# Turning the softmax weights of the queries by DMA transposes in place of TensorE transposes

## The chip, the cores and the metric

The kernel runs on one core of a Trainium2 chip. The time is the device time of one execution in microseconds, as the median of several runs; shorter is better. TensorE, VectorE (DVE), ScalarE (ACT), GpSimd (POOL) and the DMA engines work side by side, each following its own list of instructions, and wait for one another on semaphores. SP (SyncE) issues the kernel's DMAs.

## The reference

```python
def _attn_ref(q, k, v, agents):
    scale = 1.0 / np.sqrt(q.shape[-1])
    def sm(a, b):
        s = scale * (a @ b.transpose(0, 2, 1))
        s = s - s.max(-1, keepdims=True)
        e = np.exp(s)
        return e / (e.sum(-1, keepdims=True) + 1e-09)
    agent_v = sm(agents, k) @ v
    return sm(q, agents) @ agent_v          # x, then the layer:

def _moe_ref(x, w_in, w_out, alpha):
    h = x @ w_in
    g = np.maximum(h, 0.0) + alpha * np.minimum(h, 0.0)
    return g @ w_out
```

`q`, `k` and `v` are 2 x 12480 x 128 in float32, `agents` is 2 x 49 x 128, `w_in` 128 x 2048, `w_out` 2048 x 128.

## The kernel before

Setup computes the attention of the 49 agents over the keys and values of batch 0, and folds it with `w_in` into matrices `M_a`, `M_r` (and `L_a`, `L_b` for the linear part of the activation), all float16 in high and low parts. After that, each query needs only its 49 softmax weights: `h` is those weights times the folded matrix.

The main loop goes over 52 chunks of 480 queries, two chunks (`half` 0 and 1) in a body; `n` is the chunk. The bodies come in kinds: KEYS, TOP, VALUES, SUMS, MIX, MIX_REST do pieces of the same setup for batch 1 between the chunks of batch 0, PLAIN bodies (the second half of the run) do nothing beside the chunks. The order of each engine's instructions is written out by hand.

The softmax of chunk n+1 is computed while chunk n is in the second layer. Its parts are:

- TensorE, `query_score` (L501), four float32 matmuls in `second_layer(6)` of the chunk before; DVE, `query_shift`; ACT, `query_exp`; DVE, `query_sum`, `query_norm` (L1096).
- `stack` is 120 queries x 4 tiles x 128 in float16. Columns 0 to 48 are the weights rounded (`query_hi`, ACT L850), the next 49 what the rounding lost (`query_lo`, DVE L1100), the last 30 a copy of part of the high ones (`query_again`, POOL L354).
- `query_turn` (TensorE L517): four transposes, 120 x 128 to 128 x 120, into the PSUM bank `SMALL`; they stand behind the two `linear` matmuls of chunk n (L551). `query_out` (ACT L854) copies the result to `PT`, 128 x 480.
- `spread` (SP L259): rows 0 to 31 of `PT` are copied to rows 32 to 63, 64 to 95 and 96 to 127 of `PR` by three DMAs of 30 KB.

Both buffers have a half for each parity of n. A chunk then is, on TensorE: `tiles(p)` (L524), two matmuls `PT` x `M_a` of 480 columns for each of eight pairs p of feature tiles; `rest_of_quad(q)` (L531), four matmuls of 32 rows on `PT` and `PR` for each two pairs; and `second_layer(p)` (L541), six matmuls. ACT makes `r_hi` (`relu_hi`, L862) of each pair from the PSUM, DVE makes `r_lo` (`relu_lo`, L1105). `tiles(p)` waits for the low part of the pair that had its PSUM slot before (three slots). `tiles(0)`, `tiles(1)` and `rest_of_quad(0)` of chunk n+1 stand before `second_layer(6)` of chunk n, and `rest_of_quad(0)` is the first that waits for `PR`:

```python
tiles(0, 1 - half, nb)
pe.wait_ge(lo_ready, g + 7)
tiles(1, 1 - half, nb)

pe.wait_ge(q_spread, 48 * n + 96)
rest_of_quad(0, 1 - half, nb)
```

SP's list in one chunk of a PLAIN body: the load of `q` for chunk n+2 (L276), the three copies into `PR`, the store of `y` (L295). In KEYS and VALUES bodies a load of 512 or 768 KB into `kv_s` (L280, L289) stands before the copies.

Of the kernel before, what the change touches and what calls it, by code (L numbers as in the profile page):

```python
# [6 lines left out]
F16 = mybir.dt.float16  # L7
ALU = mybir.AluOpType
# [6 lines left out]
T = 120  # L15
CHUNK = 4 * T
CHUNKS = B * N // CHUNK
KT = 128
# [22 lines left out]
def build(nc, kT, kTail, vP, vS, vTail, qT, agT, w_inT, w_out, alpha_col, out):  # L41
    ctx = ExitStack()
    with ctx:
# [8 lines left out]
        ident16 = sb("ident16", [128, 128], F16)  # L52
# [85 lines left out]
        def slot(p):  # L138
# [14 lines left out]
        consts, pool_step, dve_step = sem("consts"), sem("pool_step"), sem("dve_step")  # L153
# [17 lines left out]
        q_scored, q_maxed, q_shifted, q_exped, q_summed, q_dened, q_reced, q_normed, q_hi, q_lo, q_turned, q_ready, q_dup, q_spread = (  # L171
            sem(x) for x in ("q_scored", "q_maxed", "q_shifted", "q_exped", "q_summed", "q_dened", "q_reced",
                             "q_normed", "q_hi", "q_lo", "q_turned", "q_ready", "q_dup", "q_spread"))
# [48 lines left out]
        def _(sp):  # L222
# [38 lines left out]
            spread(0, 0)  # L261
# [8 lines left out]
            def body(i, b, kind, last):  # L270
                for half in range(2):
                    n = 2 * i + half
                    if not last:

                        sp.wait_ge(q_scored, n + 1)
                        sp.dma_start(q_s[:, half, :], qT[n + 2]).then_inc(in_q[half], 16)  # L276
                    if kind == KEYS and (not isinstance(n, int) or n + 2 + EARLY <= FULL):

                        sp.wait_ge(k_scored, n + (FULL + EARLY + 2))
                        sp.dma_start(kv_s[:, half, :], kT[1, n + (EARLY + 1)]).then_inc(in_k[half], 16)  # L280
                    if kind == TOP:

                        sp.wait_ge(v_used, FULL + 1)
                        sp.dma_start(second_s[:, half * SECOND * C:(half + 1) * SECOND * C],
                                     vS[half]).then_inc(in_second[half], 16)
                    if kind == VALUES and (not isinstance(n, int) or n + 2 - FIRST_VALUES < SECONDS):

                        sp.wait_ge(v_used, n + (FULL + 2 - FIRST_VALUES))
                        sp.dma_start(second_s[:, half * SECOND * C:(half + 1) * SECOND * C],  # L289
                                     vS[n + (2 - FIRST_VALUES)]).then_inc(in_second[half], 16)  # L290
                    if not (last and half == 1):
                        spread(n + 1, 1 - half)
# [9 lines left out]
        def _(pool):  # L302
            pool.memset(agents[:, B * A:128], 0.0).then_inc(consts, 1)
            pool.memset(ident[:, :], 0.0).then_inc(pool_step, 1)
            pool.memset(ident16[:, :], 0.0).then_inc(pool_step, 1)
# [5 lines left out]
            pool.wait_ge(pool_step, 3)  # L311
            for m in (ident, ident16):
                pool.affine_select(out=m[:, :], in_=m[:, :], compare_op=ALU.not_equal, fill=1.0, base=0,
                                   pattern=[[-1, 128]], channel_multiplier=1).then_inc(consts, 1)
# [3 lines left out]
            steps = 3  # L318
# [23 lines left out]
            pool.wait_ge(consts, 8)  # L342
# [8 lines left out]
            def query_again(n):  # L351

                pool.wait_ge(q_hi, n + 1)
                pool.tensor_tensor(stack[:, :, 2 * A:128], stack[:, :, REST:A],  # L354
                                   ones[0:T, 0:4 * SPARE].rearrange("p (t a) -> p t a", a=SPARE), ALU.mult).then_inc(q_dup, 1)
# [29 lines left out]
        def _(pe):  # L385
# [124 lines left out]
            def query_turn(n):  # L510

                pe.wait_ge(q_hi, n + 1)
                pe.wait_ge(q_lo, n + 1)
                pe.wait_ge(q_dup, n + 1)
                turned = ps[:, SMALL, :].bitcast(F16)
                for t in range(4):
                    mm = pe.transpose(turned[:, t * T:(t + 1) * T], stack[:, t, :], ident16[0:T, 0:T])  # L517
                mm.then_inc(q_turned, 1)


            def tiles(p, half, b):
                for u in range(2):
                    f = 128 * (2 * p + u)
                    pe.matmul(ps[:, 2 * slot(p) + u, 0:CHUNK], M_a[:, b, f:f + 128], PT[:, half, :],  # L524
                              start=True, stop=False)


            def rest_of_quad(q, half, b):
                for u in range(4):
                    src = PT if u == 0 else PR  # L530
                    mm = pe.matmul(ps[:, 2 * slot(2 * q + u // 2) + u % 2, 0:CHUNK],  # L531
                                   M_r[32 * u:32 * u + 32, b, q * 128:(q + 1) * 128],
                                   src[32 * u:32 * u + 32, half, :], start=False, stop=True)
                mm.then_inc(h_ready, 1)
# [14 lines left out]
            def linear(half, b):  # L549
                for w, end in ((L_a, False), (L_b, True)):  # L550
                    mm = pe.matmul(ps[:, 2 * LIN_SLOT, 0:CHUNK], w[:, b, :], PT[:, half, :], start=not end, stop=end)  # L551
                mm.then_inc(lin_ready, 1)
# [5 lines left out]
            for m in range(1, FULL + 1):  # L558
                first_scores(m)
                if m == 7:  # L560

                    pe.wait_ge(consts, 8)
                    relu_max_row()
                if m == 8:
                    relu_max_everywhere()
# [26 lines left out]
            query_turn(0)  # L592
# [8 lines left out]
            pe.wait_ge(q_ready, 1)  # L601
# [21 lines left out]
            pe.wait_ge(m_low, 1)  # L623
            tiles(0, 0, 0)
# [11 lines left out]
            def body(i, b, kind, last):  # L636
                for half in range(2):
# [85 lines left out]
                    if ahead:  # L723

                        if keys:
                            pe.wait_ge(k_saved, n + (FULL + EARLY + 2))
                        if kind == TOP and half == 1:
                            pe.wait_ge(b_shift, 2)
                        if kind == VALUES:
                            pe.wait_ge(av_added, n + (1 - FIRST_VALUES))  # L730
                        if kind == SUMS and half == 0:
                            pe.wait_ge(av_added, SECONDS + 1)
                        if kind == SUMS and half == 1:
                            pe.wait_ge(b_dened, 2)
                        if kind == MIX:
                            pe.wait_ge(m_low, 5 + 2 * half)
                        if kind == MIX_REST and half == 0:
                            pe.wait_ge(r_low, 2)
                        query_turn(n + 1)

# [7 lines left out]
                    if ahead:  # L748
                        pe.wait_ge(q_ready, n + 2)
                    if kind == TOP and half == 0:  # L750
                        key_max_rows(1, SMALL)
                    if kind == SUMS and half == 1:
                        value_sums(1, SMALL)
                    if kind == MIX:
                        mix(1, 2 * half + 1, SMALL)
                    if kind == MIX_REST and half == 0:
                        mix_linear(1, SMALL)
                    second_layer(5, half)

                    if ahead:  # L760
                        pe.wait_ge(lin_saved, n + 1)
                        if kind == MIX_REST and half == 1:
                            pe.wait_ge(m_low, 8)
                            pe.wait_ge(r_low, 2)
                            pe.wait_ge(l_low, 2)
                        tiles(0, 1 - half, nb)
# [8 lines left out]
                    else:  # L775
                        pe.wait_ge(in_q[half], 16 * i + 32)

                        if kind == TOP and half == 0:
                            pe.wait_ge(b_diag, 2)
                        if kind == SUMS and half == 1:  # L780
                            pe.wait_ge(b_vmax, 2)
# [18 lines left out]
        def _(act):  # L800
# [47 lines left out]
            def query_hi(n):  # L848
                act.wait_ge(q_normed, n + 1)
                act.activation(stack[:, :, 0:A], q_p[:, :, :], ACT.Copy).then_inc(q_hi, 1)  # L850
# [18 lines left out]
            for m in range(FULL + 1):  # L869
# [11 lines left out]
                if m == 11:  # L881
                    query_out(0, 0)
# [15 lines left out]
            def body(i, b, kind, last):  # L898
                for half in range(2):
# [20 lines left out]
                    if ahead:  # L920
                        query_out(n + 1, 1 - half)
# [27 lines left out]
        def _(dve):  # L949
# [148 lines left out]
            def query_lo(n):  # L1098
                dve.wait_ge(q_hi, n + 1)
                dve.tensor_tensor(stack[:, :, A:2 * A], q_p[:, :, :], stack[:, :, 0:A], ALU.subtract).then_inc(q_lo, 1)  # L1100
# [12 lines left out]
            dve.wait_ge(consts, 8)  # L1113
# [169 lines left out]
```

## Time and profile before

| | us |
|---|---|
| median of 3 runs | 944.13 (944.05 to 944.71) |
| the profiled execution | 944.28 |
| its span in the profile | 942.8 |

| engine | busy, share of the span | instructions |
|---|---|---|
| TensorE matmuls | 925.7 us (98%) | 5850 |
| TensorE weight loads | 499.9 (53%) | 5850 |
| DVE | 635.4 (67%) | 926 |
| ACT | 540.4 (57%) | 746 |
| POOL | 109.1 (12%) | 142 |

The span is what the profiler's records cover, the time is the whole execution, 1.5 us more. A TensorE matmul is listed with its own duration, 0.37 us for 480 columns, and the next starts 0.2 us after it, since they are pipelined: the distance between starts is what one costs. The granted clock is 1.00 at TensorE's full 2.4 GHz and 0.50 at 1.2 GHz.

### The profile page before, as it was taken

Reading aid. Unit: us, or ns where it says so; the run is one execution under the profiler, and the core shown is the slowest. Engines: PE = TensorE matmul, PEld = TensorE weight load, DVE = VectorE, ACT = ScalarE, POOL = GpSimd, SP = SyncE. Lnnn points to the kernel's source line nnn. Section 1 sums busy time; section 2 is a strip of 40 time slices with the busy share of each in tenths; the row PEclk is TensorE's granted clock in tenths of the full one; section 3 lists DMA queues with packets and bytes.
Section 4 is the critical chain, followed back from the end, with each engine's and each line's share of the span. In section 5 each row is a group of like instructions: output and inputs, shape, how many; then the busy total and the mean of one; then the engine's idle time right before and its main releaser. Section 6 shows DMA issues by size and latency. Waiting matters only on the chain.

```text
span 942.8 us, 16143 instructions
## 1 busy us (share of the span) xinstructions
PE 925.7 (98%) x5850; PEld 499.9 (53%) x5850; DVE 635.4 (67%) x926; ACT 540.4 (57%) x746; POOL 109.1 (12%) x142
## 2 busy tenths in 40 slices
PE   7899999999999999999999999999999999999998
PEld 7784555555546556554444444444444444444443
DVE  4567666666767767767776676766666666666664
ACT  2236565565565565565656666666666666656564
POOL 6220100101001001001001010101010101010101
PEclk9799999999999999999999999999999999999999
DMA  8650221221212311201101110101111110101010
GB/s 296 262 189 28 62 77 51 77 64 48 80 63 70 102 62 66 72 29 46 29 26 47 29 46 29 46 29 45 30 43 32 36 39 32 42 26 47 26 37 24
DMA packets 29922, 58.55 MB, mean 62 GB/s; under 512 B 5248, under 2 KB 24000, under 8 KB 29632
## 3 DMA queue, kind: packets, MB, share of 16 engines
q1 hardware_dynamic: 29600, 58.03, 18.9%
q8 instruction: 23, 0.38, 0.2%
q14 instruction: 11, 0.09, 0.0%
q10 hardware_dynamic: 288, 0.06, 0.0%
HBM read 40.49 MB, written 12.78 MB: 57 GB/s over the span
## 4 chain that ended last, share of the span: by engine, by line
PE 94%; DVE 2%; issue 2%; DMA 1%; ACT 1%; SPq 0%; POOLq 0%; ACTq 0%
PE ps L541 54%; PE ps L524 17%; PE ps L531 7%; PE ps L501 3%; PE ps L551 2%; PE ps L388 2%; PE ps L694 2%; PE ps L688 1%; PE ps L517 1%; PE ps L464 1%; DMA kv_s<-kT 1%; PE ps L412 1%; PE ps L482 1%; DVE r_lo L1105 0%; PE ps L419 0%
## 5 line engine op out<-in xcount | busy, mean ns | idle before, releaser
L1105 DVE SCALAR_TENSOR_TENSOR r_lo<-ps,r_hi 128x960 f16<-128x960 f32 x416 | 466.5, 1153 | 259.4 <-ACT r_hi L862 256.7
L862 ACT ACTIVATE r_hi<-ps 128x960 f16<-128x960 f32 x416 | 386.3, 967 | 154.3 <-PE ps L531 149.2
L541 PE MATMUL ps<-r_hi,w_hi 128*128 128x480 f16 x832 | 252.1, 369 | 0.3 <-DVE M_a L1057 0.3
L541 PE MATMUL ps<-r_hi,w_lo 128*128 128x480 f16 x832 | 248.1, 366 | 0.0
L541 PE MATMUL ps<-r_lo,w_hi 128*128 128x480 f16 x832 | 240.7, 366 | 0.0
L524 PE MATMUL ps<-PT,M_a 128*128 128x480 f16 x832 | 204.0, 366 | 0.7 <-DVE r_lo L1105 0.7
L373 POOL TENSOR_TENSOR y<-y_relu,y_lin 128x480 f32<-128x480 f32 x52 | 62.4, 1200 | 627.4 <-issue 377.3
L541 PEld LDWEIGHTS ps<-r_hi,w_lo 128*128 128x128 f16 x832 | 91.4, 111 | 68.5
L541 PEld LDWEIGHTS ps<-r_lo,w_hi 128*128 128x128 f16 x832 | 85.4, 106 | 71.0
L541 PEld LDWEIGHTS ps<-r_hi,w_hi 128*128 128x128 f16 x832 | 77.1, 106 | 86.0 <-issue 41.9
L524 PEld LDWEIGHTS ps<-PT,M_a 128*128 128x128 f16 x832 | 75.6, 98 | 80.1 <-DVE r_lo L1105 16.8
L531 PE MATMUL ps<-PR,M_r 32*128 32x480 f16 x624 | 78.6, 371 | 0.0
L531 PE MATMUL ps<-PT,M_r 32*128 32x480 f16 x208 | 77.3, 372 | 0.2 <-DMA PR<-PT 0.2
L501 PEld LDWEIGHTS ps<-agents,q_s 128*120 128x120 f32 x416 | 71.2, 187 | 3.9
L943 ACT ACTIVATE y_relu<-ps,out_unscale 128x480 f32<-128x480 f32 x52 | 34.4, 662 | 65.2 <-PE ps L541 65.2
L854 ACT ACTIVATE PT<-ps 128x480 f16<-128x480 f16 x52 | 29.7, 571 | 64.7 <-PE ps L517 64.7
L501 PE MATMUL ps<-agents,q_s 128*120 128x49 f32 x416 | 65.0, 241 | 0.0
L531 PEld LDWEIGHTS ps<-PT,M_r 32*128 32x128 f16 x208 | 18.9, 91 | 82.9 <-issue 81.4
L850 ACT ACTIVATE stack<-q_p 120x196 f16<-120x196 f32 x52 | 19.4, 373 | 60.4 <-DVE q_p L1096 60.4
L354 POOL TENSOR_TENSOR stack<-stack,ones 120x120 f16<-120x120 f16 x52 | 20.9, 402 | 179.2 <-ACT stack L850 179.2
L926 ACT ACTIVATE y_lin<-ps,lin_unscale 128x480 f32<-128x480 f32 x52 | 34.1, 656 | 1.1 <-PE ps L551 1.1
L694 PEld LDWEIGHTS ps<-S,kv_s 128*128 128x128 f32 x192 | 33.2, 190 | 1.4
(146 smaller groups left out, 599.6 us busy)
## 6 DMA issues: line engine op xcount, KB each, us to landing
q_s<-qT SPq DMA_DIRECT2D x52, 240.0 KB, 2.6
out<-y SPq DMA_DIRECT2D x52, 240.0 KB, 2.0
kv_s<-kT SPq DMA_DIRECT2D x24, 512.0 KB, 4.4
kv_s<-vP SPq DMA_DIRECT2D x12, 512.0 KB, 6.7
kv_s<-vS SPq DMA_DIRECT2D x8, 768.0 KB, 4.4
PR<-PT SPq DMA_DIRECT2D x156, 30.0 KB, 1.9
w_lin<-w_out SPq DMA_DIRECT2D x1, 1024.0 KB, 6.8
w_inT_s<-w_inT SPq DMA_DIRECT2D x1, 1024.0 KB, 5.6
```

Source lines behind the costliest of these rows:

```text
L354: pool.tensor_tensor(stack[:, :, 2 * A:128], stack[:, :, REST:A], ones[0:T, 0:4 * SPARE].rearrange("p (t a) -> p t a", a=SPARE), ALU.mult) ...
L373: pool.tensor_tensor(y[:, half, :], y_relu[:, half, :], y_lin[:, half, :], ALU.add).then_inc(y_ready, 1)
L501: return pe.matmul(ps[0:T, SMALL, t * A:(t + 1) * A], q_s[:, half, t * T:(t + 1) * T], agents[:, b * A:(b + 1) * A], start=True, stop=True)
L524: pe.matmul(ps[:, 2 * slot(p) + u, 0:CHUNK], M_a[:, b, f:f + 128], PT[:, half, :], start=True, stop=False)
L531: mm = pe.matmul(ps[:, 2 * slot(2 * q + u // 2) + u % 2, 0:CHUNK], M_r[32 * u:32 * u + 32, b, q * 128:(q + 1) * 128], src[32 * u:32 * u + ...
L541: mm = pe.matmul(ps[:, OUT, 0:CHUNK], w[:, 2 * p + u, :], r[:, s, u, :], start=(p == 0 and u == 0 and k == 0), stop=(p == PAIRS - 1 and u ...
L694: mm = pe.matmul(ps[:, SMALL, 0:A], second_s[:, at:at + C], S[:, 1, SECOND * n + (t + 2 - SECOND * FIRST_VALUES), :], start=(t == 0), stop ...
L854: act.activation(PT[:, half, :], ps[:, SMALL, :].bitcast(F16)[:, 0:CHUNK], ACT.Copy).then_inc(q_ready, 1)
L862: act.activation(r_hi[:, p % RING, :, :], ps[:, at:at + 2, 0:CHUNK], ACT.Relu).then_inc(hi_ready, 1)
L926: act.activation(y_lin[:, half, :], ps[:, 2 * LIN_SLOT, 0:CHUNK], ACT.Copy, scale=lin_unscale[:, b, :]).then_inc(lin_saved, 1)
L943: act.activation(y_relu[:, half, :], ps[:, OUT, 0:CHUNK], ACT.Copy, scale=out_unscale[:, b, :]).then_inc(relu_saved, 1)
L1105: dve.scalar_tensor_tensor(out=r_lo[:, p % RING, :, :], in0=ps[:, at:at + 2, 0:CHUNK], scalar=0.0, in1=r_hi[:, p % RING, :, :], op0=ALU.ma ...
```

## The change

The four TensorE transposes of a chunk, their PSUM output and the copy to `PT` on ACT are gone. SP issues four DMA transposes of 128 x 128 from `stack` to `PT`, waits for them to land, and then issues the three copies to `PR`. For this `stack` gets 128 partitions (the last 8 are zeroed once, by one memset on the DVE), and `PT` and `PR` get 512 columns for each half, of which 120 in each 128 are used; the matmuls on them read them in four runs. The float16 identity is gone from POOL's list. The waits that stood before `query_turn` for the PSUM bank move to where the bank is used next. TensorE waits for the transposes before `tiles(0)` of the next chunk.

```diff
-        stack = sb("stack", [T, 4, 128], F16)
-        PT = sb("PT", [128, 2, CHUNK], F16)
-        PR = sb("PR", [128, 2, CHUNK], F16)
+        stack = sb("stack", [WIDE, 4, 128], F16)
+        PT = sb("PT", [128, 2, 4 * WIDE], F16)
+        PR = sb("PR", [128, 2, 4 * WIDE], F16)
...
-            def spread(n, half):
-
-                sp.wait_ge(q_ready, n + 1)
+            def turn(n, half):
+
+                sp.wait_ge(stack_zero, 1)
+                sp.wait_ge(q_hi, n + 1)
+                sp.wait_ge(q_dup, n + 1)
+                sp.wait_ge(q_lo, n + 1)
+                for t in range(4):
+                    sp.dma_start(PT[:, half, t * WIDE:(t + 1) * WIDE], stack[:, t, :], transpose=True).then_inc(q_turned, 16)
+
+                sp.wait_ge(q_turned, 64 * n + 64)
                 for g in range(32, 128, 32):
                     sp.dma_start(PR[g:g + 32, half, :], PT[0:32, half, :]).then_inc(q_spread, 16)
...
-            def query_turn(n):
-
-                pe.wait_ge(q_hi, n + 1)
-                pe.wait_ge(q_lo, n + 1)
-                pe.wait_ge(q_dup, n + 1)
-                turned = ps[:, SMALL, :].bitcast(F16)
-                for t in range(4):
-                    mm = pe.transpose(turned[:, t * T:(t + 1) * T], stack[:, t, :], ident16[0:T, 0:T])
-                mm.then_inc(q_turned, 1)
+            def tokens(x, half):
+                return x[:, half, :].rearrange("p (t n) -> p t n", n=WIDE)[:, :, 0:T]
...
-                    pe.matmul(ps[:, 2 * slot(p) + u, 0:CHUNK], M_a[:, b, f:f + 128], PT[:, half, :],
+                    pe.matmul(by_tile(ps[:, 2 * slot(p) + u, 0:CHUNK]), M_a[:, b, f:f + 128], tokens(PT, half),
                               start=True, stop=False)
...
+                        pe.wait_ge(q_turned, 64 * n + 128)
+                        tiles(0, 1 - half, nb)
+                        pe.wait_ge(lo_ready, g + 7)
+                        tiles(1, 1 - half, nb)
+
+                        pe.wait_ge(q_spread, 48 * n + 96)
+                        rest_of_quad(0, 1 - half, nb)
...
-            def query_out(n, half):
-                act.wait_ge(q_turned, n + 1)
-                act.activation(PT[:, half, :], ps[:, SMALL, :].bitcast(F16)[:, 0:CHUNK], ACT.Copy).then_inc(q_ready, 1)
...
+            dve.memset(stack[:, :, :], 0.0).then_inc(stack_zero, 1)
```

In the loop over the PLAIN bodies, TensorE's list between `linear` and `second_layer(4)` was this; L551 is `linear`, L517 the transposes, L524 `tiles(6)` and `tiles(7)`, L531 `rest_of_quad(3)`:

```order
L551 MATMUL ps<-PT,L_b 128x480
L512 REGISTER_ALU
L517 MATMUL ps<-ident,stack 128x120 [waits q_dup,q_lo,q_hi]
L517 MATMUL ps<-ident,stack 128x120 x3
L741 REGISTER_ALU
L524 MATMUL ps<-PT,M_a 128x480 [waits lo_ready]
L524 MATMUL ps<-PT,M_a 128x480
L743 REGISTER_ALU
L524 MATMUL ps<-PT,M_a 128x480 [waits lo_ready]
L524 MATMUL ps<-PT,M_a 128x480
L531 MATMUL ps<-PT,M_r 128x480
```

and is this in the changed kernel, whose lines are numbered five higher or more (L556 is `linear`, L529 `tiles`, L536 `rest_of_quad`):

```order
L556 MATMUL ps<-PT,L_b 128x480
L729 REGISTER_ALU
L529 MATMUL ps<-PT,M_a 128x480 [waits lo_ready]
L529 MATMUL ps<-PT,M_a 128x480
L731 REGISTER_ALU
L529 MATMUL ps<-PT,M_a 128x480 [waits lo_ready]
L529 MATMUL ps<-PT,M_a 128x480
L536 MATMUL ps<-PT,M_r 128x480
```

The transposes and their wait for `stack` are gone from between `linear` and `tiles(6)`; nothing else moved there. SP's list for one chunk of the same loop was this:

```order
L276 ISA [waits q_scored]
L276 DMA q_s<-qT 128x480
L259 DMA PR<-PT 32x480 [waits q_ready]
L259 DMA PR<-PT 32x480 x2
L295 ISA [waits y_ready]
L295 DMA out<-y 128x480
```

and is now this:

```order
L286 ISA [waits q_scored]
L286 DMA q_s<-qT 128x480
L265 DMA_TRANSPOSE PT<-stack 128x128 [waits q_dup,q_lo,q_hi,stack_zero]
L265 DMA_TRANSPOSE PT<-stack 128x128 x3
L267 ISA
L269 DMA PR<-PT 32x512 [waits q_turned]
L269 DMA PR<-PT 32x512 x2
L305 ISA [waits y_ready]
L305 DMA out<-y 128x480
```

Four transposes and a wait for them stand ahead of the copies, which began on ACT's copy before.

## Rows read from the trace of the kernel before

**Rows 1.** Busy time by stretch: stretch, its length, each engine's, PEclk, DMA share.

```profile
698.94:714.82 15.88, 15.88 (x95) 7.60 (x95) 10.77 (x16) 9.74 (x13) 1.60 (x2) 1.00 0.12 37
```

**Rows 2.** Waits of TensorE, whole run: who, for whom, us in total, times, longest.

```profile
PE ps L531 <- DMA PR<-PT: 0.2, 1, 0.2
```

**Rows 3.** Timeline, last stage: start, us, instructions; then idle before and its releaser.

```profile
698.94 0.37 PE L531 MATMUL ps<-PT,M_r 32*128 32x480 f16 x1
...
707.93 0.35 DVE L1100 TENSOR_TENSOR stack<-q_p,stack 120x196 f16<-120x196 f32 x1
```

**Rows 4.** Timeline, same chunk, from the end of `stack` to `rest_of_quad(0)`.

```profile
708.37 2.22 DVE L1105 SCALAR_TENSOR_TENSOR r_lo<-ps,r_hi 128x960 f16<-128x960 f32 x2
...
710.01 0.38 PE L517 MATMUL ps<-ident,stack 120*128 120x120 f16 x4
...
710.23 1.00 PE L524 MATMUL ps<-PT,M_a 128*128 128x480 f16 x4
710.43 0.57 ACT L854 ACTIVATE PT<-ps 128x480 f16<-128x480 f16 x1 [1.23 <-PE ps L517]
710.64 0.11 PEld L524 LDWEIGHTS ps<-PT,M_a 128*128 128x128 f16 x2 [0.32 <-DVE r_lo L1105]
...
711.02 1.78 SPq L259 DMA_DIRECT2D PR<-PT  x3
...
713.92 0.97 PE L524 MATMUL ps<-PT,M_a 128*128 128x480 f16 x4
...
714.82 0.37 PE L531 MATMUL ps<-PT,M_r 32*128 32x480 f16 x1
```

**Rows 5.** The copies into `PR`: issue min/median/max ns, first and last start; landing.

```profile
L259 SPq DMA_DIRECT2D PR<-PT x156: 512/590/1503, 60.6 to 918.7; - x156
...
DMA to landing us min/median/max: 1.8/1.9/2.8
```

**Rows 6.** Timeline, a chunk of the KEYS stage with a slow issue.

```profile
226.03 2.71 SPq L259 DMA_DIRECT2D PR<-PT  x3
...
230.06 0.09 PEld L531 LDWEIGHTS ps<-PT,M_r 32*128 32x128 f16 x1 [0.67 <-DMA PR<-PT]
```

**Rows 7.** Timeline, last stage: the load of `q` on the SP queue.

```profile
705.30 0.35 SPq L276 DMA_DIRECT2D q_s<-qT  x1
```

**Rows 8.** Timeline of KEYS, VALUES and SUMS: the end of `stack`, `rest_of_quad(0)`.

```profile
136.11 0.35 DVE L1100 TENSOR_TENSOR stack<-q_p,stack 120x196 f16<-120x196 f32 x1
...
144.24 0.37 PE L531 MATMUL ps<-PT,M_r 32*128 32x480 f16 x1
...
325.76 0.35 DVE L1100 TENSOR_TENSOR stack<-q_p,stack 120x196 f16<-120x196 f32 x1
325.77 0.33 SPq L289 DMA_DIRECT2D kv_s<-vS  x1
...
334.31 0.37 PE L531 MATMUL ps<-PT,M_r 32*128 32x480 f16 x1
...
432.08 0.35 DVE L1100 TENSOR_TENSOR stack<-q_p,stack 120x196 f16<-120x196 f32 x1
...
439.23 0.37 PE L531 MATMUL ps<-PT,M_r 32*128 32x480 f16 x1
```

**Rows 9.** The value loads of 768 KB (L289): time to landing.

```profile
DMA to landing us min/median/max: 4.1/4.3/4.4
```

**Rows 10.** Busy time by stretch around two pauses of TensorE in the setup.

```profile
19.50:21.50 2.00, 0.06 (x2) 0.05 (x2) 2.00 (x2) 0.50 (x1) 0.00 (x0) 1.00 0.89 297
21.50:24.90 3.40, 3.40 (x15) 2.98 (x16) 0.97 (x3) 0.00 (x0) 0.00 (x0) 0.50 0.40 154
...
62.90:64.30 1.40, 0.15 (x3) 0.07 (x1) 1.18 (x3) 0.00 (x0) 0.00 (x0) 1.00 0.47 116
65.90:69.30 3.40, 3.40 (x23) 3.04 (x19) 1.48 (x5) 0.52 (x2) 0.00 (x0) 0.50 0.98 355
```

More of the change, by code:

```diff
@@ L291, in body @@
                     if not (last and half == 1):
-                        spread(n + 1, 1 - half)
+                        turn(n + 1, 1 - half)
                     sp.wait_ge(y_ready, n + 1)
@@ L310, in _ @@
             pool.memset(av_acc[:, :], 0.0).then_inc(consts, 1)
[L311 to L314, printed above, removed]
+            pool.wait_ge(pool_step, 2)
+            pool.affine_select(out=ident[:, :], in_=ident[:, :], compare_op=ALU.not_equal, fill=1.0, base=0,
+                               pattern=[[-1, 128]], channel_multiplier=1).then_inc(consts, 1)
             pool.affine_select(out=gate[:, :], in_=gate[:, :], compare_op=ALU.is_ge, fill=0.0, base=-2 * A,
                                pattern=[[0, 1]], channel_multiplier=1).then_inc(consts, 1)
-            steps = 3
+            steps = 2
             def then(instruction):
@@ L353, in query_again @@
                 pool.wait_ge(q_hi, n + 1)
[L354 removed]
+                pool.tensor_tensor(stack[0:T, :, 2 * A:128], stack[0:T, :, REST:A],
                                    ones[0:T, 0:4 * SPARE].rearrange("p (t a) -> p t a", a=SPARE), ALU.mult).then_inc(q_dup, 1)
@@ L530, in rest_of_quad @@
                     src = PT if u == 0 else PR
-                    mm = pe.matmul(ps[:, 2 * slot(2 * q + u // 2) + u % 2, 0:CHUNK],
+                    mm = pe.matmul(by_tile(ps[:, 2 * slot(2 * q + u // 2) + u % 2, 0:CHUNK]),
                                    M_r[32 * u:32 * u + 32, b, q * 128:(q + 1) * 128],
-                                   src[32 * u:32 * u + 32, half, :], start=False, stop=True)
+                                   tokens(src[32 * u:32 * u + 32, :, :], half), start=False, stop=True)
                 mm.then_inc(h_ready, 1)
@@ L550, in linear @@
                 for w, end in ((L_a, False), (L_b, True)):
-                    mm = pe.matmul(ps[:, 2 * LIN_SLOT, 0:CHUNK], w[:, b, :], PT[:, half, :], start=not end, stop=end)
+                    mm = pe.matmul(by_tile(ps[:, 2 * LIN_SLOT, 0:CHUNK]), w[:, b, :], tokens(PT, half), start=not end,
+                                   stop=end)
                 mm.then_inc(lin_ready, 1)
@@ L722, in body @@
                     linear(half, b)
[L723 to L739, printed above, removed]
                     pe.wait_ge(lo_ready, g + 5)
@@ L746, in body @@
                     second_layer(4, half)
-                    if ahead:
-                        pe.wait_ge(q_ready, n + 2)
                     if kind == TOP and half == 0:
+                        pe.wait_ge(k_saved, 2 * FULL + 2)
                         key_max_rows(1, SMALL)
                     if kind == SUMS and half == 1:
+                        pe.wait_ge(b_dened, 2)
                         value_sums(1, SMALL)
                     if kind == MIX:
+                        pe.wait_ge(m_low, 5 + 2 * half)
                         mix(1, 2 * half + 1, SMALL)
                     if kind == MIX_REST and half == 0:
+                        pe.wait_ge(r_low, 2)
                         mix_linear(1, SMALL)
@@ L776, in body @@
                         pe.wait_ge(in_q[half], 16 * i + 32)
+                        if kind == KEYS:
+                            pe.wait_ge(k_saved, n + (FULL + EARLY + 2))
                         if kind == TOP and half == 0:
                             pe.wait_ge(b_diag, 2)
+                        if kind == TOP and half == 1:
+                            pe.wait_ge(b_shift, 2)
+                        if kind == VALUES:
+                            pe.wait_ge(av_added, n + (1 - FIRST_VALUES))
+                        if kind == SUMS and half == 0:
+                            pe.wait_ge(av_added, SECONDS + 1)
                         if kind == SUMS and half == 1:
@@ L1099, in query_lo @@
                 dve.wait_ge(q_hi, n + 1)
-                dve.tensor_tensor(stack[:, :, A:2 * A], q_p[:, :, :], stack[:, :, 0:A], ALU.subtract).then_inc(q_lo, 1)
+                dve.tensor_tensor(stack[0:T, :, A:2 * A], q_p[:, :, :], stack[0:T, :, 0:A], ALU.subtract).then_inc(q_lo, 1)
             def relu_lo(g, p):
```

29 lines of the change are left out of this document (13 added, 16 removed).

## The prediction

> **What bounds the kernel now.** I read the busy shares by stretch first. Over one chunk of the last stage TensorE is busy for all of its 15.88 us, at the full granted clock [rows 1], and in the whole run it waits for the copies in `PR` just once, for 0.2 us [rows 2]. So any time that TensorE gets back is worth something, and any time for which it is made to wait is a loss. What decides is therefore the two things that the change touches: the TensorE work of the transposes, and the slack of the path that brings the turned weights to TensorE.
>
> For that path I followed one chunk of the last stage in order of time. `rest_of_quad(0)` of one chunk starts at 698.94, the score matmuls for the next one follow, then its softmax, woven on the DVE between the low parts of this chunk; the last piece of `stack` ends at 707.93 + 0.35 = 708.28 [rows 3]. From 698.94 to there is **9.34 us**. All of it follows from `rest_of_quad(0)` through work that the change leaves alone, so this length stays. From 708.28 to the next `rest_of_quad(0)` at 714.82 [rows 4] is **6.54 us**: the budget of everything between `stack` and `PR`. The sum of the two is the period of 15.88 us.
>
> **What the change removes.** Four transposes on TensorE: from 710.01 to the next matmul at 710.23 [rows 4], 0.22 us per chunk, 52 x 0.22 = 11.4 us if all of it came back (the 0.38 us of the four overlap with their neighbours, so the distance of starts is the price). It does not come back. Two matmuls further, the third `L524` of the group is `tiles(7)`, which needs the fourth low part of the DVE, and the DVE's two operations run 708.37 to 708.37 + 2.22 = 710.59, with the weight load at 710.64 already waiting for them [rows 4]. They follow from `rest_of_quad(2)` through ScalarE (`relu_hi`), not from the transposes, which come later on TensorE. Without transposes TensorE stands there 0.2 us earlier and waits until 710.64 all the same. What is left is the 0.03 us by which that group of four takes 1.00 instead of the 0.97 of its like at 713.92 [rows 4]. I take the removal at **0 us**, with 0.03 x 52 = 2 us as its most in the last stage and, in the others, at most the 0.1 or so between these times. The PSUM copy was 0.57 us on ScalarE beside TensorE's work [rows 4], a gain of 0 by itself.
>
> The wider buffers (512 columns in place of 480 in each copy), the single DVE memset at the start and the one memset and one select fewer on GpSimd I take at 0: TensorE's first long wait ends at 21.5 [rows 10] and is for `w_col`, long after them. The matmuls read `PT` in four runs of 120 columns with a gap; no row shows such a read, it is the same count of columns, and I take 0. If each run cost a few ns on the 8 or so matmuls of the 9.34 us, that is under 0.2 us per chunk, inside the range below.
>
> **What the change adds.** Before, the path from `stack` to `PR` was: turn and copy, with `PT` ready at 711.00, then three copies issued from 711.02 [rows 4]. The issue of one takes 0.52 to 0.59 us, it lands 1.9 us after its issue began [rows 5]; the third starts 1.19 us after the first (1.78 - 0.59). So `PR` is there at 711.02 + 1.19 + 1.9 = 714.11 against a need at 714.82: 0.7 us of slack. That the landing is rightly read shows where an issue was slow: three issues took 2.71 us from 226.03, the third began at 226.03 + 2.71 - 0.59 = 228.15, + 1.9 = 230.05, and TensorE's load is released at 230.06 [rows 6].
>
> Now the SP queue issues four transposes after `stack`, waits until the last has landed, and only then issues the three copies. Two DMAs thus stand in series where before there was one. With an issue price i and a landing l of a transpose, the path is
>
> W = 0.02 + 3i + l + 0.02 + 1.19 + 1.9 + 0.04 = 3.17 + 3i + l,
>
> where 0.02 is the SP's start after its release (711.00 to 711.02) and 0.04 TensorE's start after a landing, rounded up. If W is over a chunk's budget, the excess is TensorE idle time, and the period is 9.34 + W. Behind the waiting SP stands only the store of `y`, released some 9 us later, so nothing else is queued behind that wait; behind TensorE's wait stands everything.
>
> No row shows a transposing DMA. The bounds: i not under the 0.35 us of a plain load of 128 rows, not over the 1.503 us of the slowest issue of a copy; l from 1.8 to 2.8 us, the extremes of the copies [rows 5, 7]. The nearest row is the plain copy within the SBUF, 0.59 and 1.9. A transpose has four times its rows, and spreads elements of two bytes over partitions, so I hold that it costs more than this and not less; I take the middle of the bounds, **i = 0.93, l = 2.3, W = 8.26 us**.
>
> The budgets of the other stages, from the end of `stack` to `rest_of_quad(0)` [rows 8]: chunks with a key piece 144.24 - 136.46 = 7.78 (9 like it); with values 334.31 - 326.11 = 8.20 (9 like it; there a 768 KB load is issued at 325.77, 0.34 us ahead of the transposes, and lands after 4.3 us [rows 9], so they may queue behind it; with 3i + l = 5.1 they end after it anyway); seven chunks at the seams between 6.8 and 7.8, mean 7.15, of which the shortest kind is 439.23 - 432.43 = 6.80; and the last stage's 6.54, 26 times. Together 51; the first chunk's turn lies in the setup, where the copies were issued at 60.6 [rows 5], well ahead of the loop.
>
> Sum: 26 x (8.26 - 6.54) = 44.7; 7 x (8.26 - 7.15) = 7.8; 9 x 0.48 = 4.3; 9 x 0.06 = 0.5; together **57 us**, all of it TensorE waiting for `PR`. The profiled execution took 944.28 us (the median of the runs is 944.13, so the two can be taken as one), which gives **1001 us**. By the same formula the nearest row's prices (W = 6.84) give 26 x 0.30 = 8, so 952 us; the upper bounds (W = 10.47) give 102 + 23 + 24 + 20 = 169, so 1114 us; the lower bounds (W = 6.02) give no wait at all.
>
> The Trainium skill weighs in on both sides. Its page "Advanced Engine Details and Errata" (X-Bar Transpose (TRN2)) says that transposing DMAs are as fast as regular ones; by that it would be the 952 us case. Its page "VectorE: DVE Perf Modes" (The three transpose paths) gives 1309 ns for a 128x128 transpose by DMA; an estimate with that as i and 2.3 as l gives W = 9.4 and some 1060 us. No row here tells between them.
>
> **The rivals.** *A. The DMAs are cheap, the path fits (not slower).* It decides at W = 6.54: with l = 1.9 that needs i under 0.49, so a transpose that issues faster than the plain copy, at most like the 0.35 us load. For it: such an issue exists in the trace, for a load [rows 7]. Against: all copies within the SBUF took at least 0.51. Then only the gain remains, which the DVE holds to 0 to 4 us: 940 to 944 us. If the DVE did not hold it, it would be 933 us; the row at 710.64 [rows 4] speaks against that.
>
> *B. The waits bring TensorE's clock down.* After TensorE had stood still for 1.94 us in 19.50 to 21.50, its granted clock was 0.5, 1.2 GHz, for the next 3.4 us; after a pause of 1.25 us at 63 to 64.3 the same came over 65.9 to 69.3 [rows 10]. Such a stretch costs half its length, 1.7 us. In the forecast TensorE pauses for 1.7 us in each chunk of the last stage. 33 chunks with it (26 and 7) would add 56 us, all 51 would add 87: 1057 to 1088 us. Against it: around those two pauses TensorE ran small float32 matmuls, while in the last stage dense float16 work would stand on both sides of each pause, as nowhere in this trace. That pauses lower the clock is also what the Trainium skill says ("TensorE: Matmul & The Clock Gate", on oscillation in real kernels), and the trace agrees that it can happen.
>
> *C. The transposes are dearer than every bound here*, since 2-byte elements are moved one by one: beyond 1114 us, each further us of W costs 51.
>
> That the transposes stay on TensorE is no rival: in the order of the changed kernel they are gone from the engine and stand in the SP queue.
>
> **How the numbers follow.** Forecast (W over the budget, clock full, up to 1114): 0.70, point 1001. B: 0.12. C: 0.05. A: 0.13, of which same 0.08 and faster 0.05. A change of about 0.2% (1.9 us) is what can be told from none. Slower is 0.70 + 0.12 + 0.05 = 0.87. The range goes from the nearest row's 952, less 4 for a gain at `tiles(7)`, that is 948, up to the bounds' 1114: it leaves out A, C and little of B, somewhat under 0.2.
>
> **What would show it.** Right: in the last stage a period of 17.6 us; TensorE idle 1.7 us before `rest_of_quad(0)`, released by the copies into `PR`; SP waiting for the transposes; issues of about 0.9 us each; `tiles(7)` waiting 0.2 us for `r_lo`. No `L524` waits for `PT` itself, as the transposes are to land 5.1 us after `stack` and `tiles(0)` stands at about 5.4. Wrong: a period of 15.7 (A without the DVE), TensorE's clock below full in the last stage (B), or matmuls on `PT` longer than 0.37 us.

## The result and the profile after

The changed kernel takes **1110.85 us** (median of 4 runs, 1108.26 to 1113.56) against 944.09 of the kernel before (4 runs): a ratio of 1.177, 95% interval 1.173 to 1.180. It is slower, as forecast, and inside the range; but the point of 1001 us stood for a loss of 57 us, and the loss is 167 us, about three times that. The profiled execution took 1108.89 us, its span is 1107.2.

The line of TensorE on the page after, and its waits over the whole run (who, for whom, us in total, times, longest), which answer to [rows 2]:

```profile
PE 977.6 (88%) x5642; PEld 509.8 (46%) x5642; DVE 635.7 (57%) x927; ACT 516.2 (47%) x694; POOL 108.8 (10%) x140
```

```profile
PE ps L536 <- DMA PR<-PT: 95.6, 51, 3.3
...
PE ps L529 <- DMA PT<-stack: 14.4, 31, 0.8
```

TensorE stood still for 0.2 us for `PR` before; now it does in each of the 51 chunks that are turned in the loop, 95.6 us in all, and for `PT` 14.4 us more. That is 110 us. The matmuls were busy for 925.7 us before and for 977.6 now, though there are 208 fewer of them: 52 us more. Both are lost time, and the second is not a wait: most of it is the clock, as the rows below show.

One chunk of the last stage, in order of time, from one `rest_of_quad(0)` (L536) to the next; these rows answer to [rows 3] and [rows 4] (start, us, instructions; idle before and its releaser):

```profile
880.95 0.37 PE L536 MATMUL ps<-PT,M_r 32*128 32x480 f16 x1 [2.14 <-DMA PR<-PT]
...
883.54 1.00 PE L546 MATMUL ps<-r_hi,w_hi 128*128 128x480 f16 x2
...
884.34 1.00 PE L546 MATMUL ps<-r_hi,w_lo 128*128 128x480 f16 x2
...
887.20 0.58 PE L546 MATMUL ps<-r_hi,w_hi 128*128 128x480 f16 x2
...
891.62 0.35 DVE L1092 TENSOR_TENSOR stack<-q_p,stack 120x196 f16<-120x196 f32 x1
...
892.07 4.95 SPq L265 DMA_TRANSPOSE PT<-stack  x4
...
893.71 1.21 PE L529 MATMUL ps<-PT,M_a 128*128 128x480 f16 x4
...
894.34 0.11 PEld L529 LDWEIGHTS ps<-PT,M_a 128*128 128x128 f16 x2 [0.53 <-DVE r_lo L1097]
...
898.21 1.81 SPq L269 DMA_DIRECT2D PR<-PT  x3
...
898.24 0.98 PE L529 MATMUL ps<-PT,M_a 128*128 128x480 f16 x4 [0.47 <-DMA PT<-stack]
...
901.33 0.37 PE L536 MATMUL ps<-PT,M_r 32*128 32x480 f16 x1 [2.10 <-DMA PR<-PT]
```

The period is 901.33 - 880.95 = 20.38 us, where it was 15.88. From the end of `stack` (891.97) to `rest_of_quad(0)` it is 9.36 us; that was 6.54. The other piece, from `rest_of_quad(0)` to the end of `stack`, is 11.02 us and was 9.34, and here nothing waits for a DMA. Two matmuls of the second layer take 1.00 us from 883.54 on and 0.58 from 887.20 on: the clock. The busy times by stretch (stretch, length, each engine's, PEclk, DMA share), beside [rows 1]:

```profile
880.95:901.33 20.38, 17.74 (x91) 7.80 (x92) 10.77 (x15) 9.28 (x12) 1.60 (x2) 0.92 0.13 35
882.53:885.94 3.41, 3.41 (x11) 1.38 (x10) 2.79 (x4) 0.77 (x1) 0.00 (x0) 0.51 0.00 0
```

For 3.4 us, from 1.6 us after the pause on, TensorE's granted clock is half, 1.2 GHz, and the chunk loses 11.02 - 9.34 = 1.68 us there. Of the 26 chunks of the last stage 23 look like this, with periods of 20.34 us and up, and 3 keep the full clock and have 18.6 to 18.7, which is 9.36 + 9.34; outside that stage four chunks have the fall.

The DMAs, beside [rows 5] (issue min/median/max in ns, first and last start; landing):

```profile
L265 SPq DMA_TRANSPOSE PT<-stack x208: 1107/1232/1892, 54.1 to 1077.6; - x104
...
DMA to landing us min/median/max: 2.3/2.4/4.6
```

A transpose keeps the SP queue for 1.23 us, twice the 0.59 of a plain copy, and lands 2.4 us after its issue began.

Both parts in one sum, on the profiled executions (1108.89 - 944.28 = 164.6 us): with W = 9.36 in the prediction's formula the waits come to 26 x 2.82 + 7 x 2.21 + 9 x 1.58 + 9 x 1.16 = 113 us; the clock to 27 x 1.67 = 45 us; 6 us remain, of which a few slow issues make some 3 (in the last chunk W is 10.8).

### The profile page after: what moved, and what is told of

It is laid out like the page before. It is cut to its first block, busy times and chain, and to the rows that moved or that the text cites. A ratio compares the mean times of both kernels' runs of the same rounds, so it can differ in the third digit from the quotient of the medians.

```text
span 1107.2 us, 15981 instructions
## 1 busy us (share of the span) xinstructions
PE 977.6 (88%) x5642; PEld 509.8 (46%) x5642; DVE 635.7 (57%) x927; ACT 516.2 (47%) x694; POOL 108.8 (10%) x140
## 4 chain that ended last, share of the span: by engine, by line
PE 33%; SPq 22%; DMA 21%; DVE 14%; issue 5%; ACT 4%; POOLq 0%; ACTq 0%
PE ps L546 17%; SPq L265 17%; DMA PT<-stack 11%; DMA PR<-PT 9%; DVE r_lo L1097 7%; SPq L269 5%; ACT r_hi L858 4%; PE ps L529 4%; PE ps L509 4%; PE ps L536 3%; PE ps L396 2%; DVE stack L1092 1%; PE ps L700 1%; DVE q_sum L1080 1%; PE ps L472 1%
## 5 line engine op out<-in xcount | busy, mean ns | idle before, releaser
L546 PE MATMUL ps<-r_hi,w_hi 128*128 128x480 f16 x832 | 264.9, 385 | 0.3 <-DVE M_a L1049 0.3
L546 PE MATMUL ps<-r_hi,w_lo 128*128 128x480 f16 x832 | 263.5, 385 | 0.0
L546 PE MATMUL ps<-r_lo,w_hi 128*128 128x480 f16 x832 | 254.2, 384 | 0.0
L529 PE MATMUL ps<-PT,M_a 128*128 128x480 f16 x832 | 211.8, 367 | 17.5 <-DMA PT<-stack 14.4
L536 PE MATMUL ps<-PT,M_r 32*128 32x480 f16 x208 | 77.6, 373 | 95.6 <-DMA PR<-PT 95.6
L529 PEld LDWEIGHTS ps<-PT,M_a 128*128 128x128 f16 x832 | 74.8, 99 | 125.1 <-DVE r_lo L1097 28.0
L546 PEld LDWEIGHTS ps<-r_hi,w_lo 128*128 128x128 f16 x832 | 97.0, 117 | 74.5 <-issue 10.3
L546 PEld LDWEIGHTS ps<-r_lo,w_hi 128*128 128x128 f16 x832 | 90.2, 112 | 74.5 <-issue 6.2
L546 PEld LDWEIGHTS ps<-r_hi,w_hi 128*128 128x128 f16 x832 | 80.6, 110 | 94.3 <-issue 58.5
L536 PEld LDWEIGHTS ps<-PT,M_r 32*128 32x128 f16 x208 | 18.8, 91 | 181.7 <-DMA PR<-PT 119.3
L509 PEld LDWEIGHTS ps<-agents,q_s 128*120 128x120 f32 x416 | 88.1, 228 | 7.6
L536 PE MATMUL ps<-PR,M_r 32*128 32x480 f16 x624 | 79.0, 373 | 0.0
L509 PE MATMUL ps<-agents,q_s 128*120 128x49 f32 x416 | 77.5, 278 | 0.0
L694 PEld LDWEIGHTS ps<-agents,kv_s 128*128 128x128 f32 x176 | 30.9, 191 | 1.1
```

Of the source, the lines that this page charges most:

```text
L509: return pe.matmul(ps[0:T, SMALL, t * A:(t + 1) * A], q_s[:, half, t * T:(t + 1) * T], agents[:, b * A:(b + 1) * A], start=True, stop=True)
L529: pe.matmul(by_tile(ps[:, 2 * slot(p) + u, 0:CHUNK]), M_a[:, b, f:f + 128], tokens(PT, half), start=True, stop=False)
L536: mm = pe.matmul(by_tile(ps[:, 2 * slot(2 * q + u // 2) + u % 2, 0:CHUNK]), M_r[32 * u:32 * u + 32, b, q * 128:(q + 1) * 128], tokens(src[ ...
L546: mm = pe.matmul(ps[:, OUT, 0:CHUNK], w[:, 2 * p + u, :], r[:, s, u, :], start=(p == 0 and u == 0 and k == 0), stop=(p == PAIRS - 1 and u ...
```

## The experiments

The theory at this point: (1) only the length of the path from `stack` to `PR` makes TensorE wait, and the issues of the four transposes make it long; (2) TensorE's pauses bring its clock down, and that is 45 of the 165 us; (3) the 0.22 us of the TensorE transposes would not come back even if the waits were gone, since the DVE's low part holds `tiles(7)`. The rivals are named with each run.

### Plain copies in place of the transposes

```diff
-                    sp.dma_start(PT[:, half, t * WIDE:(t + 1) * WIDE], stack[:, t, :], transpose=True).then_inc(q_turned, 16)
+                    sp.dma_start(PT[:, half, t * WIDE:(t + 1) * WIDE], stack[:, t, :]).then_inc(q_turned, 16)
```

> The changed kernel with four plain copies of the same tiles in place of the four DMA transposes (PT then holds untransposed data, so the output is not the reference's); every wait stays. Theory (the issue price of a transpose on the SP queue, 1.24 us each, is what lengthens the path from stack to PR): issues fall to 0.59 us, landing to 1.9, the path from 9.36 to about 6.9 us, TensorE waits some 0.3 us per chunk of the last stage, its clock stays full: about 952 us. Rival 1 (two DMA steps in series cost this much whatever they are): near 1100. Rival 2 (the clock falls because of the missing TensorE transposes, not because of the pause): the path is short but the clock still falls in most chunks, about 995.

Measured: 956.45 us (ratio 1.013, 1.011 to 1.015). The SP queue and the wait at `rest_of_quad(0)` in the last stage:

```profile
810.87 2.45 SPq L265 DMA_DIRECT2D PT<-stack  x4
814.62 1.82 SPq L269 DMA_DIRECT2D PR<-PT  x3
```

```profile
801.43 0.37 PE L536 MATMUL ps<-PT,M_r 32*128 32x480 f16 x1 [0.38 <-DMA PR<-PT]
...
817.76 0.37 PE L536 MATMUL ps<-PT,M_r 32*128 32x480 f16 x1 [0.39 <-DMA PR<-PT]
```

Four issues take 2.45 us where the transposes took 4.95, and the period is 817.76 - 801.43 = 16.33. Two DMA steps in series cost 12 us; that the first of them is made of transposes costs the other 155, with the clock that falls behind the longer pauses. In the loop of this run the clock is full.

### Half of the transposes

```diff
-                for t in range(4):
+                for t in range(2):
                     sp.dma_start(PT[:, half, t * WIDE:(t + 1) * WIDE], stack[:, t, :], transpose=True).then_inc(q_turned, 16)
 
-                sp.wait_ge(q_turned, 64 * n + 64)
+                sp.wait_ge(q_turned, 32 * n + 32)
```

TensorE's waits for the transposes are halved in the same way, and the DVE zeroes `PT` once at the start.

> The changed kernel with two transposes per chunk in place of four (the other half of PT stays zero, so the output is not the reference's). Theory: two issues of 1.24 us less, the path is 9.36 - 2.48 = 6.88 us, the clock stays full: about 953 us. Rival (the price is in the landing of a transpose, or in the wait, not in the issue of each): the path stays over 8 us, and the time over 1000.

Measured: 953.52 us (ratio 1.010, 1.008 to 1.012).

```profile
809.89 2.40 SPq L265 DMA_TRANSPOSE PT<-stack  x2
813.48 1.81 SPq L269 DMA_DIRECT2D PR<-PT  x3
```

```profile
816.62 0.37 PE L536 MATMUL ps<-PT,M_r 32*128 32x480 f16 x1 [0.22 <-DMA PR<-PT]
```

From the first issue of the transposes to the first of the copies is now 813.48 - 809.89 = 3.59 us; with four it was 898.21 - 892.07 = 6.14. Two issues of 1.2 us less shorten the path by 2.55: the price is in the issue of each, not in the landing or the wait as such.

### Work in the pause

```diff
                         tiles(1, 1 - half, nb)
+                        if kind == PLAIN:
+                            for _ in range(14):
+                                pe.matmul(ps[:, SMALL, 200:500], w_hi[:, 0, :], M_a[:, 1, 0:300], start=True, stop=True,
+                                          skip_group_check=True)
```

> The changed kernel with 14 added matmuls of 300 columns into unused columns of the PSUM bank SMALL, in each chunk of the last stage, between tiles(1) and the wait for PR; the output is not changed. They fill about 1.8 of the 2.1 us of pause. Theory (the pauses bring the clock down, and each fall costs 1.67 us in about 23 chunks of the last stage): the period of the last stage is 18.7 in place of 20.4 us, the clock full there: about 1072 us. Rival 1 (the clock falls whatever TensorE does in the pause): 1111 us. Rival 2 (added work delays rest_of_quad(0)): over 1111.

Measured: 1072.68 us (ratio 1.136, 1.133 to 1.139), 38 us less than the changed kernel, with more work in it. The filler and the wait behind it, then two stretches of the last stage in this run:

```profile
933.89 1.95 PE L763 MATMUL ps<-M_a,w_hi 128*128 128x300 f16 x14
...
936.20 0.37 PE L536 MATMUL ps<-PT,M_r 32*128 32x480 f16 x1 [0.36 <-DMA PR<-PT]
...
954.89 0.37 PE L536 MATMUL ps<-PT,M_r 32*128 32x480 f16 x1 [0.32 <-DMA PR<-PT]
```

```profile
900.00:950.00 50.00, 48.14 (x279) 22.88 (x278) 30.15 (x44) 26.30 (x36) 4.79 (x6) 1.00 0.14 41
950.00:1000.00 50.00, 47.45 (x281) 23.58 (x279) 28.33 (x41) 23.88 (x31) 4.39 (x5) 1.00 0.13 37
```

and the same two of the changed kernel:

```profile
900.00:950.00 50.00, 43.35 (x232) 21.05 (x232) 26.52 (x40) 23.13 (x30) 4.40 (x5) 0.93 0.13 37
950.00:1000.00 50.00, 43.47 (x222) 19.93 (x218) 27.31 (x36) 23.25 (x30) 3.60 (x5) 0.93 0.13 36
```

The clock goes from 0.93 to 1.00, and the path to `PR` is as long as before: the period is 954.89 - 936.20 = 18.69 us, as in the chunks of the changed kernel that kept the clock. So the pause is what brings the clock down, and 38 us is what that cost in the last stage: 23 chunks by 1.67.

### The same path made of plain copies

```diff
+                for t in range(4):
+                    sp.dma_start(again[:, t * WIDE:(t + 1) * WIDE], stack[:, t, :]).then_inc(q_again, 16)
                 for t in range(4):
-                    sp.dma_start(PT[:, half, t * WIDE:(t + 1) * WIDE], stack[:, t, :], transpose=True).then_inc(q_turned, 16)
+                    sp.dma_start(PT[:, half, t * WIDE:(t + 1) * WIDE], stack[:, t, :]).then_inc(q_turned, 16)
```

> The run plain with four more plain copies of the stack, into a buffer that nobody reads, issued ahead of the four copies into PT (the output is not the reference's). No transposing DMA is in it. By the formula the path from stack to PR is 3.2 + 7 x 0.61 + 1.9 = 9.4 us, as with the transposes. Theory (only the length of the path counts, for the waits and for the clock): the same 1105 to 1115 us, the granted clock at half for 3.4 us in most chunks of the last stage. Rival (the fall of the clock belongs to the transposing DMAs): the waits as expected, the clock full: 1060 to 1070 us.

Measured: 1131.7 us (ratio 1.200, 1.197 to 1.204): 17 us above the theory's 1105 to 1115 and 21 above the changed kernel, and far from the rival's.

```profile
826.62 2.45 SPq L267 DMA_DIRECT2D again<-stack  x4
829.12 2.53 SPq L269 DMA_DIRECT2D PT<-stack  x4
832.92 1.83 SPq L274 DMA_DIRECT2D PR<-PT  x3
```

```profile
832.95 0.98 PE L534 MATMUL ps<-PT,M_a 128*128 128x480 f16 x4 [0.62 <-DMA PT<-stack]
...
836.03 0.56 PE L541 MATMUL ps<-PT,M_r 32*128 32x480 f16 x1 [2.10 <-DMA PR<-PT]
```

```profile
900.00:950.00 50.00, 44.40 (x230) 21.15 (x230) 27.62 (x42) 23.26 (x32) 4.79 (x6) 0.92 0.16 44
```

From the first issue to the copies it is 6.30 us, 0.16 more than with the transposes, and the first pause 0.62 in place of 0.47. The clock falls without any transposing DMA. That a path of nearly the same length costs 21 us more lies partly in its 0.16 us (51 x 0.16 = 8 us), partly in the clock, which falls in all 26 chunks of the last stage here and in more chunks ahead of it. The mean granted clock is 0.939 over a span of 1127.5 us, and 0.949 over 1107.2 in the changed kernel, so that 0.061 x 1127.5 - 0.051 x 1107.2 = 12 us more are lost to it. Why it falls in more chunks was not tried.

This run also has pauses that leave the clock up. In the key stage TensorE waits for `PR` alone, 1.7 us in each of the six chunks from 156.23 to 269.39 us, and the clock stays full there (the wait of one chunk, then the stretch of all six, with PEclk 1.00):

```profile
212.91 0.37 PE L541 MATMUL ps<-PT,M_r 32*128 32x480 f16 x1 [1.71 <-DMA PR<-PT]
```

```profile
156.23:269.39 113.16, 102.70 (x636) 56.18 (x638) 70.11 (x97) 57.91 (x78) 9.60 (x12) 1.00 0.24 69
```

In the changed kernel these chunks have pauses of 1.5 to 1.6 us, also at full clock.

### TensorE never waits for the DMAs

TensorE reads the first chunk's weights from buffers of their own, and all DMAs are issued as before; ScalarE waits for a chunk's copies before it writes `stack` anew, which TensorE's reads assured before:

```diff
-                    pe.matmul(by_tile(ps[:, 2 * slot(p) + u, 0:CHUNK]), M_a[:, b, f:f + 128], tokens(PT, half),
+                    pe.matmul(by_tile(ps[:, 2 * slot(p) + u, 0:CHUNK]), M_a[:, b, f:f + 128], tokens(PT0, half),
...
-                        pe.wait_ge(q_turned, 64 * n + 128)
...
-                        pe.wait_ge(q_spread, 48 * n + 96)
```

> The changed kernel, all transposes and copies issued as before, but TensorE reads the weights of the first chunk for every chunk, from buffers of their own, and so never waits for the DMAs of the loop (the output is not the reference's). Theory (the DVE's low parts hold tiles(7), so TensorE gets back almost nothing of the 0.22 us of transposes per chunk): 940 to 944 us, with a wait of about 0.2 us for r_lo before tiles(7) in each chunk of the last stage. Rival (TensorE's work is the only bound): 944 - 11 = 933 us, and no such wait. If the reads of PT in four runs cost something, the matmuls of tiles stand further apart than 0.203 us.

Measured: 943.05 us (10 runs; ratio 0.9986, 0.9977 to 0.9996). The chunk around `tiles(7)`:

```profile
802.72 1.21 PE L532 MATMUL ps<-PT,M_a 128*128 128x480 f16 x4
...
806.62 0.97 PE L532 MATMUL ps<-PT,M_a 128*128 128x480 f16 x4
```

```profile
803.35 0.11 PEld L532 LDWEIGHTS ps<-PT,M_a 128*128 128x128 f16 x2 [0.53 <-DVE r_lo L1100]
```

The group with `tiles(7)` takes 1.21 us, 0.24 more than its like, and the load waits for `r_lo`: 0.21 us longer than in [rows 4]. The 0.22 us of the transposes have become this wait. The other group, also read from four runs of 120 columns, takes 0.97 us as before, so that read costs nothing. And the DMAs, all in flight, disturb nobody.

### Two matmuls ahead of the wait

```diff
+                    second_layer(4, half, part=(0,))
                     pe.wait_ge(lo_ready, g + 6)
                     tiles(7, half, b)
                     rest_of_quad(3, half, b)
-                    second_layer(4, half)
+                    second_layer(4, half, part=(1, 2))
```

This on top of the run free, and alone on the kernel before:

> The run free (TensorE reads the first chunk's weights throughout and never waits for the DMAs of the loop; the output is not the reference's), with the first two matmuls of second_layer(4) moved ahead of tiles(7). Theory (the DVE's low part of pair 5 is what kept the 0.22 us of the transposes per chunk from coming back in free, where a wait of that length stood before tiles(7)): the two matmuls fill it, the period of the last stage falls from 15.86 to 15.66 us, and the time from 943 to about 933 us. Rival (the time in free is set by something else, such as the reads of PT in four runs): 943 us again.

> The kernel before, with only the move of the two matmuls of second_layer(4) ahead of tiles(7). TensorE had no wait there but 0.03 us, as its transposes filled the time: 942 to 944 us, no difference to speak of. If the move by itself saves time, it is below 940.

Measured: 932.08 us (ratio 0.987, 0.986 to 0.989) with it on free, 943.99 us (11 runs; ratio 1.000, 0.999 to 1.001) on the kernel before. The move is worth nothing by itself and 11 us once the transposes are off TensorE. Work taken away and the wait behind it have to go together.

### The turn one chunk earlier

The whole softmax of the queries runs one chunk further ahead; the transposes of chunk n+2 wait until TensorE has read the same half of `PT` for the last time in chunk n:

```diff
-                sp.wait_ge(q_hi, n + 1)
                 sp.wait_ge(q_dup, n + 1)
                 sp.wait_ge(q_lo, n + 1)
+                if not (isinstance(n, int) and n < 2):
+                    sp.wait_ge(pt_free, n + 1)
...
-                    if not (last and half == 1):
-                        turn(n + 1, 1 - half)
+                    if not last:
+                        turn(n + 2, half)
```

and likewise `query_shift`, `query_exp`, `query_sum`, `query_norm`, `query_hi`, `query_lo` and `query_again` of n+2 for n+1, and the scores and the load of chunk n+3 for n+2. ACT waits for the transposes before it writes `stack` anew.

> The changed kernel with the whole softmax of the queries, its DMA transposes and copies one chunk earlier against their use: chunk n+2 is turned while chunk n runs, once TensorE has done with the same half of PT; the output is the reference's. Theory (only the length of the path from stack to PR, 9.4 us against a budget of 6.5, made the change slow, and with it the clock): no wait for PT or PR in any chunk, full clock, and the time of the run free, 943 us, with 1 to 2 us more in the setup: 942 to 946. Rival (the DMAs disturb other work, or the SP queue becomes late): over 950.

> The run deep with the first two matmuls of second_layer(4) ahead of tiles(7); the output is the reference's. Theory: both gains of the change come out, 933 to 937 us, about 1% under the kernel before. Rival (the wait for r_lo only moves elsewhere): 943 us.

Measured: deep 948.7 us (9 runs; ratio 1.004, 1.003 to 1.005), above the expected 946; deep_early 939.01 us (5 runs; ratio 0.995, 0.993 to 0.996), above the expected 937. No chunk of the loop waits for `PT` or `PR` any more. What was missed lies in the setup: the first chunk of deep took 24.67 us between the first two `rest_of_quad(0)`, 18.33 before, for this:

```profile
80.21 0.36 DVE L1099 TENSOR_TENSOR q_e<-ps,q_top 120x196 f32<-120x196 f32 x1
...
80.83 0.56 PE L556 MATMUL ps<-r_hi,w_hi 128*128 128x480 f16 x1 [2.91 <-DVE q_e L1099]
```

The third softmax's shift stood behind a low part on the DVE, and TensorE waited 2.91 us for it before its first `second_layer`; the matmuls after it run at half clock (0.56 us). So the score matmuls and the shift were moved forward:

```diff
             rest_of_quad(0, 0, 0)
+            pe.wait_ge(q_shifted, 2)
+            pe.wait_ge(in_q[0], 32)
+            for t in range(4):
+                mm = query_score(t, 0, 0)
...
             relu_lo(0, 0)
+            query_shift(2)
             mixed_low(0, 1, F_BANK[1])
```

> The run deep_early with the scores of chunk 2 and their shift placed earlier in the setup: the score matmuls ahead of mix(0,1), the DVE's shift ahead of the next low part. In deep_early TensorE stood still for 2.9 us before the first second_layer, waiting for that shift, and at half clock for some us after it; the first chunk took 24.7 us in the run deep where it took 18.3 before. Theory: the first chunk takes about 18 to 19 us, the rest is unchanged, 932 to 935 us; the output is the reference's. Rival (the setup has no room for a second softmax): 937 to 939 us again.

Measured: **933.2 us** (ratio 0.988, 0.986 to 0.990), 1.2% faster than the kernel before. TensorE's time over 100 us of the last stage, and SP's list over one chunk:

```profile
700.00:800.00 100.00, 100.00 (x576) 47.04 (x575) 68.48 (x95) 59.02 (x78) 9.98 (x13) 1.00 0.16 45
```

```profile
846.23 4.96 SPq L271 DMA_TRANSPOSE PT<-stack  x4
852.36 1.82 SPq L275 DMA_DIRECT2D PR<-PT  x3
854.50 0.36 SPq L314 DMA_DIRECT2D out<-y  x1
855.07 0.36 SPq L295 DMA_DIRECT2D q_s<-qT  x1
861.87 4.95 SPq L271 DMA_TRANSPOSE PT<-stack  x4
```

The transposes are as slow as ever, 4.96 us of issue, and the period is 861.87 - 846.23 = 15.64 us. Now that their result is used a period later, nobody waits for them. The copies' issue ends at 854.18, 0.3 us ahead of the store of `y`; whether the SP queue would be the next limit was not tried. The kernel has both changes in it, the earlier turn and the two matmuls ahead of the wait: deep, with the turn alone, was 5 us slower than the kernel before, through its longer first chunk.

## Why the prediction was wrong

**What bounds the kernel and the budget of 6.54 us:** right. Plain, two and free all came out within 5 us of what these lengths gave. Of the 9.34 us ahead of `stack` the prediction said "so this length stays". It did in the chunks at full clock; in 23 of the 26 of the last stage it was 11.0 us. That is the second step that failed, below.

**What the change removes, 0 us:** right, and for the reason given: free shows the wait at `tiles(7)`, and free_early its end. Without that row the forecast for a hidden path would have been 933, not 943.

**What the change adds, the formula W = 3.17 + 3i + l:** right in form. With the measured 1.23 and 2.4 it gives 9.26, and the trace shows 9.36; 0.08 of the rest is SP's start, 0.10 us after the end of `stack` and not 0.02.

**The value of i was the step that failed first.** I took the middle of two bounds, 0.93, for want of a row, and it is 1.23; l was 2.3 and is 2.4. By the prediction's own sum W = 9.36 gives 113 us in place of 57. Each 0.1 us of i is 0.3 us per chunk, in 51 chunks: such a term should not have been centred, as if its error were small, but carried as the main uncertainty. The 1309 ns that the Trainium skill gives for a 128x128 transpose by DMA ("VectorE: DVE Perf Modes", The three transpose paths) is close to what an issue took here, though the page does not say that it means the issue, and the landing took 2.4 us. The Trainium skill's sentence that transposing DMAs are as fast as regular ones ("Advanced Engine Details and Errata", X-Bar Transpose (TRN2)) does not hold for issues of this size: 1.23 against the 0.59 to 0.61 us of a plain copy.

**The length of 9.34 us was the step that failed second.** It was taken as untouched, since the change leaves its work alone, and the clock was left to rival B, with 0.12, and was no term of the sum. The price of B was rightly worked out (1.7 us a time, 56 us for 33 chunks; measured 1.67 us in 27 chunks, 45 us). At the pauses of plain and two, 0.2 to 0.4 us, the clock stayed up in the loop; at those of the last stage of the changed kernel, 0.5 and 2.1 us a chunk, it fell in 23 chunks of 26. Whether it would have fallen at the pause that I forecast, one of 1.7 us in each 17.6, no run shows; the nearest rows are those of the key stage in plain8, 1.7 us in each 18.9, and there it stayed up. So the second miss may well have followed from the first. My reason against B, dense work on both sides of the pause, did not protect: fill shows that what helps is work in the pause. Both terms on the forecast, 944 + 113 + 45 = 1102, come near to 1111. What stays open is why 3 chunks of the last stage kept the clock, and what decides at pauses of about 2 us: ahead of the last stage of the changed kernel the clock fell after a single pause of 1.96 us (at 133.59), and not after two of 0.30 and 2.03 us (at 303.57).

That 1111 lies inside the stated range is partly luck: its upper end, 1114, was worked out from dearer DMAs at full clock, and not from the sum that came about.

**Rival A** was refuted by the issue price, **C** did not occur: W stayed under the upper bounds.

**The signs:** the period of 17.6 us was 20.38; the issues of 0.9 us were 1.23; the wait for `PT`, forecast as absent, was there, 0.47 us, as 3 x 1.23 + 2.4 = 6.1 us is past the place of `tiles(0)`; the wait of `tiles(7)` for `r_lo` was there as forecast. The prediction put `tiles(0)` at 5.4 us, without the 0.22 us that by its own argument do not come back; with them it is 713.92 - 708.28 = 5.64 [rows 4].

## What to carry to other kernels

Before moving a step from a busy engine to a DMA, measure the slack between its input and its use, and compare it with the whole chain: for each step in series the issues ahead of its last one, and one landing. If it doesn't fit, see whether the step can start a period earlier; here its speed then hardly mattered. The same slow transposes cost 167 us one way and, with two matmuls moved as well, are in a kernel that is 11 us faster the other way. And a forecast of repeated pauses of TensorE is incomplete without a term for the clock that they may bring down behind them.

## What was not expected of the hardware

- The issue of a DMA transpose of 128 x 128 float16 within the SBUF takes 1.11 to 1.89 us of the SP queue, median 1.23, a plain copy of the same tile 0.61 (2.45 for four); the landing differs less, 2.4 against 1.9 us.
- Pauses of 0.5 and 2.1 us in each 20.4 us, in an otherwise dense stream, bring TensorE to 1.2 GHz for 3.4 us of nearly each such period; with 1.95 us of matmuls in the longer pause it stays at 2.4 GHz (fill), and so it does with a single pause of 1.7 us in each 18.9 (plain8).
- Matmuls that read their moving operand in four runs of 120 columns take the same time as from one run of 480: 0.97 us for four, in free and before.
